# Tiles that straddle two batches take the three-pass path, and w_out2 is split earlier on GpSimd

## The chip, the cores and the metric

The kernel runs on one core of a Trainium2 chip. The metric is device time in microseconds for one execution of the whole program.

## What is computed

A packed attention feeds two feed-forward layers. In the reference, cut to what matters:

```python
# q, k, v: (8, 8, 576, 64), p: (8, 8, 32, 64)
p_packed = sm_attn(p, k, v)                  # 32 packed rows per head
x = sm_attn(q, p_packed, p_packed)           # -> (4608, 512): tokens by head features

h = x @ w_in                                 # (4608, 1024)
sm = softmax(h)
solu = h * sm
ln = (solu - mean(solu)) / sqrt(var(solu) + 1e-6) * g_ln
x = ln @ w_out                               # (4608, 512)

h = maximum(maximum(x @ w1, x @ w2), x @ w3) # (4608, 768)
out = h @ w_out2                             # (4608, 512)
```

## The kernel before

The work runs in three stages, and TensorE's instructions stand in one hand-written order.

**Attention (batches 0 to 7).** For each batch b the kernel forms two things in place of x: the attention weights of the 576 tokens over the packed rows (a, 128 rows for each of two groups of heads), and the packed values already multiplied by w_in (merged, 128 rows by 1024 for each of the two groups). From batch 2 on both are stored to DRAM by GpSimd (m_dram, a_dram; semaphores m_stored and a_stored) and come back later through SP (load_in).

**Stage one (blocks t = 0 to 8 of four tiles of 128 tokens).** Tile n = 4t + i is up(t, i): h = a^T x merged, two halves of 512 columns. 576 is 4.5 tiles, so two batches share nine tiles, and the tiles n = 4, 13, 22 and 31 straddle two batches. The even batch lies in m_even and a_even, the odd one in m_odd and a_odd, each as a pair hi and lo in the format fp32r; the product is three matmuls (PASSES: hi x lo, hi x hi, lo x hi) in `three_passes`, line 783. ScalarE writes hi (hi_in), VectorE lo (lo_in, which counts in_split). `split_after` says after which tile the halves of each batch are made: batch 3 after tile 10, batch 5 after tile 19, batch 7 after tile 28. The slots hold zeros beside the tokens of their batch, so that a straddling tile may be a sum over both. Tile 4 is computed in that way.

The straddling tiles 13, 22 and 31 are computed otherwise: SP loads both batches' merged values and the 64 tokens that each contributes, unsplit, into straddle_m and straddle_a (`load_straddle`), and up issues plain float32 matmuls (line 990), 64 columns of weights each, into the upper or the lower half of the output's partitions. These two tensors lie in the memory of w_out2_s.

A block on TensorE (solu_block) is: up(t,0), up(t,1), down(t-1,0), down(t-1,1), up(t,2), up(t,3), down(t-1,2), down(t-1,3), then four turn_h (transposes, line 1073). down is ln @ w_out, 24 matmuls each, also at line 783. VectorE takes the row maximum, the product and the moments; ScalarE the exponential and the hi parts ln_hi; VectorE writes ln_lo with four subtractions (`lo_t`, line 1574), and up(t+1, 0) waits for the first of them. `block_scale(t)` on GpSimd turns the moments of a block into scales (scale_ready); VectorE's moments of block t + 1 wait for it ahead of a reciprocal, since they overwrite its input.

GpSimd's queue also holds the preparation of the last stage's weights. `split_operands(s)`, nine of them, takes pieces of w1, w2, w3 out of weight_raw (two buffers), forms sums, splits all into hi and lo and stores them to DRAM (w_dram, semaphores w_stored). How many follow block_scale(t) is written out, for t = 0 to 7:

```python
for _ in range((0, 1, 2, 1, 2, 2, 1, 0)[t]):
```

w_out2 is split by GpSimd in three pieces (`split_w_out2`, lines 607 and 609) behind block_scale(7), once tile 31 is done (h_filled at 32), because straddle_m and straddle_a use its place until then.

**Stage two.** 4.5 double blocks of nine groups (lines 1171 and 1194) with operands from DRAM in a ring of three slots, and an output product with w_out2 (line 1203). SP issues load_slot(0) only behind store_y(7), w_stored of all nine pieces, and w_out2_split at 3.

Of the kernel before, what the change touches and what calls it, by code (L numbers as in the profile page):

```python
# [20 lines left out]
P = 128  # L21
# [12 lines left out]
DM = H * D  # L34
# [36 lines left out]
def packed_attention_ffn(nc, q, k, v, p, w_in, w_out, g_ln, w1, w2, w3, w_out2, out):  # L71
# [44 lines left out]
    ln_base = cursor[0]  # L116
    ln = place_split("ln", [P, K1, BLK])
    w_out2_s = place_split("w_out2_s", [P, K2, DM])
    straddle_m = place_at(cursor[0] - 2 * K2 * DM * 4, "straddle_m", [P, 2, QUADS, FF1])
    straddle_a = place_at(cursor[0] - 2 * K2 * DM * 4 + 2 * QUADS * FF1 * 4, "straddle_a", [P, 2, QUADS, TAIL])  # L120
    y_raw_base = cursor[0]
    y_raw = place("y_raw", [P, 2, 2, BLK])
    u_base = cursor[0]
# [120 lines left out]
    a_hi, a_low = sem("a_hi"), sem("a_low")  # L244
    m_stored, a_stored = sem("m_stored"), sem("a_stored")
    in_loaded = [sem(f"in_loaded{i}") for i in range(2)]
    straddle_loaded, w_out2_loaded = sem("straddle_loaded"), [sem(f"w_out2_loaded{i}") for i in range(2)]
    w_out2_hi, w_out2_split = sem("w_out2_hi"), sem("w_out2_split")
    in_hi, in_split = sem("in_hi"), sem("in_split")
    packed_first, packed_second = sem("packed_first"), sem("packed_second")  # L250
    gain_loaded, minus_half_ready = sem("gain_loaded"), sem("minus_half_ready")
# [34 lines left out]
    w_out_v = w_out.rearrange("(k p) n -> p k n", p=P)  # L286
    w_out2_v = w_out2.rearrange("(k p) n -> p k n", p=P)
    thirds = [w.rearrange("(k p) (m i n) -> p k m i n", p=P, m=2, n=P) for w in (w1, w2, w3)]
    def raw_operands(n):
        return weight_raw[n % 2][:, :].rearrange("p (o k n) -> p o k n", o=4, n=P)  # L290

    def raw_count(n):
        return 32 * (n // 2 + 1)

    def rows(t):
        return t.rearrange("b (h g) (p j) d -> b (g p) h (j d)", g=QUADS, j=J)
# [126 lines left out]
    with block:  # L423

        @block.sync
        def _(sp):
# [35 lines left out]
                sp.dma_start(a_s[b % 2][:, 1, :, first:first + S].bitcast(F32), a_dram[b])\  # L462
                    .then_inc(in_loaded[b % 2], 16)

            def load_straddle(q):

                if q > 1:
                    sp.wait_ge(h_filled, 9 * (q - 1) + 5)
                for x in range(2):
                    at = slice(S - TAIL, S) if x == 0 else slice(0, TAIL)  # L470
                    sp.dma_start(straddle_m[:, x, :, :], m_dram[2 * q + x]).then_inc(straddle_loaded, 16)
                    sp.dma_start(straddle_a[:, x, :, :], a_dram[2 * q + x][:, :, at]).then_inc(straddle_loaded, 16)

            load_k(0)
            load_p(0)
            load_k(1)
# [48 lines left out]

            for t in range(6):
                load_in(t + 2)
                if t == 0:
                    sp.wait_ge(m_stored, 16 * (B - 2))
                    sp.wait_ge(a_stored, 16 * (B - 2))  # L530
                    load_straddle(1)
                elif t in (3, 5):
                    load_straddle((t + 1) // 2)
                store_y(t)
                if t == 1:

                    sp.wait_ge(y_stored, 32)
                    sp.wait_ge(m_stored, 16 * (B - 2))
                    load_y(0, 0)
# [2 lines left out]

            sp.wait_ge(w_stored[0], 16 * GROUPS)
            sp.wait_ge(w_stored[1], 16 * GROUPS)
            sp.wait_ge(w_out2_split, K2 // 2)
            load_slot(0)
            sp.wait_ge(y_split, Y_PARTS)
            load_y(0, 1)
# [32 lines left out]
        def _(pool):  # L581
# [7 lines left out]
                           allow_slow_non_contiguous=True).then_inc(gain_loaded, 16)  # L589
            wait_alone(pool, gain_loaded, 16)  # L590

            def load_operands(n):
                i, w = divmod(n, 3)
                dst = weight_raw[n % 2][:, :].rearrange("p (m k n) -> p m k n", m=2, n=P)
                for m in range(2):
                    pool.dma_start(dst[:, 1 - m, :, :], thirds[w][:, :, m, i, :]).then_inc(raw_loaded[n % 2], 16)

            def load_w_out2(n):
                dst = weight_raw[n % 2][:, :].rearrange("p (k n) -> p k n", k=2)
                pool.dma_start(dst, w_out2_v[:, 2 * n:2 * n + 2, :]).then_inc(w_out2_loaded[n % 2], 16)  # L600

            def split_w_out2(n):

                hi, low = (w[:, 2 * n:2 * n + 2, :] for w in w_out2_s)
                raw = weight_raw[n % 2][:, :].rearrange("p (k n) -> p k n", k=2)
                wait_alone(pool, w_out2_loaded[n % 2], 16 * (n // 2 + 1))
                pool.tensor_scalar(hi, raw, 1.0, None, ALU.mult).then_inc(w_out2_hi, 1)
                wait_alone(pool, w_out2_hi, n + 1)
                pool.tensor_tensor(low, raw, hi.bitcast(F32), ALU.subtract).then_inc(w_out2_split, 1)

            def split_operands(s):

                n = s
                raw = raw_operands(n)
                wait_alone(pool, raw_loaded[n % 2], raw_count(n))

                def add(k, c, a, b, op, value):
                    if value:
                        pool.wait_ge(sums_step, value)
                    pool.tensor_tensor(sums[:, c, :, :], a, b, op).then_inc(sums_step, 1)  # L620

                add(0, 0, raw[:, A21], raw[:, A22], ALU.add, 4 * s)
                add(1, 2, raw[:, A11], raw[:, A21], ALU.subtract, 0)
                add(2, 1, sums[:, 0, :, :], raw[:, A11], ALU.subtract, 4 * s + 1)
                add(3, 3, raw[:, A12], sums[:, 1, :, :], ALU.subtract, 4 * s + 3)

                if s > 0:

                    pool.wait_ge(w_stored[0], 16 * s)
                pool.tensor_scalar(stage[:, 0:4, 0, :, :], raw, 1.0, None, ALU.mult).then_inc(weight_hi, 1)  # L630
                pool.wait_ge(weight_hi, n + 1)
                pool.tensor_tensor(stage[:, 0:4, 1, :, :], raw, stage[:, 0:4, 0, :, :].bitcast(F32), ALU.subtract)\
                    .then_inc(weight_split, 1)
                wait_alone(pool, weight_split, n + 1)
                pool.dma_start(w_dram[s][:, 0:4], stage[:, 0:4, :, :, :].bitcast(F32)).then_inc(w_stored[0], 16)
                if n + 2 < GROUPS:

                    load_operands(n + 2)
                pool.wait_ge(sums_step, 4 * s + 4)
                if s > 0:  # L640

                    pool.wait_ge(w_stored[1], 16 * s)
                pool.tensor_scalar(stage[:, 4:8, 0, :, :], sums[:, :, :, :], 1.0, None, ALU.mult).then_inc(sums_hi, 1)
                pool.wait_ge(sums_hi, s + 1)
                pool.tensor_tensor(stage[:, 4:8, 1, :, :], sums[:, :, :, :], stage[:, 4:8, 0, :, :].bitcast(F32),
                                   ALU.subtract).then_inc(sums_split, 1)
                pool.wait_ge(sums_split, s + 1)
                pool.dma_start(w_dram[s][:, 4:8], stage[:, 4:8, :, :, :].bitcast(F32)).then_inc(w_stored[1], 16)
# [101 lines left out]
            store_merged(B - 1)  # L750
            store_weights(B - 1)
            for n in range(2):
                load_operands(n)
            block_scale(0)
            s = 0
            for t in range(1, BLOCKS - 1):
                block_scale(t)
                if t == BLOCKS - 2:
                    for n in range(2):
                        load_w_out2(n)  # L760

                    wait_alone(pool, h_filled, 9 * 3 + 5)
                    for n in range(K2 // 2):
                        split_w_out2(n)
                        if n + 2 < K2 // 2:
                            wait_alone(pool, w_out2_split, n + 1)
                            load_w_out2(n + 2)
                for _ in range((0, 1, 2, 1, 2, 2, 1, 0)[t]):
                    split_operands(s)
                    s += 1  # L770
            block_scale(BLOCKS - 1)


        @block.tensor
        def _(pe):
# [178 lines left out]
            def up(t, i):  # L954
# [2 lines left out]
                terms = tile_terms(n)  # L957

                batch = 2 * (n // 9) + terms[-1][0]
                if n > 9 and len(terms) > 1:  # L960
                    pe.wait_ge(straddle_loaded, 64 * (n // 9))
                elif batch < 2:
                    for low_ready in m_low:
                        pe.wait_ge(low_ready, batch + 1)
                    pe.wait_ge(a_low, batch + 1)
                else:
                    pe.wait_ge(in_split, 2 * (batch - 1))
# [14 lines left out]
                else:  # L982

                    pe.wait_ge(h_used, TPB * t + i - 1)
                if n > 9 and len(terms) > 1:

                    for g in range(QUADS):
                        for w in range(WIDE):
                            for x in range(2):
                                last = pe.matmul(ps[half(x), bank + w, :], straddle_a[:, x, g, :],  # L990
                                                 straddle_m[:, x, g, w * 512:(w + 1) * 512],
                                                 start=g == 0, stop=g == QUADS - 1)
                    last.then_inc(h_filled, 1)
                    return
                three_passes([(ps[:, bank + w, :],
                               [([a_s[slot][:, e, g, at] for e in range(2)],
                                 [m_s[slot][:, e, g, w * 512:(w + 1) * 512] for e in range(2)])
# [211 lines left out]
            def outputs(t, tiles):  # L1209
# [3 lines left out]
                base = 4 * MH * t  # L1213

                pe.wait_ge(h2_split, base + parts * (MH - 1))
                if t == 0:
                    pe.wait_ge(w_out2_split, K2 // 2)
                if t < FOUR:

                    pe.wait_ge(c12_ready, GROUPS * (t + 1) - 1)  # L1220
# [788 lines left out]
```

## Time and profile before

| | |
|---|---|
| median of 3 runs | 1022.33 us (1021.81 to 1023.21) |
| profiled execution | 1022.33 us, its span 1020.5 us |
| TensorE (PE) busy | 993.5 us |
| VectorE (DVE) busy | 594.0 us |
| ScalarE (ACT) busy | 356.0 us |
| GpSimd (POOL) busy | 269.4 us |

The span is the time from the first to the last instruction in the trace. PE are matmuls, PEld loads of weights, which overlap them; SPq is SyncE's queue of DMA issues. Matmuls are pipelined: a single one is recorded as longer than the distance to the next one's start, so durations of matmuls aren't added up, and starts are compared instead. L783 is line 783 of the kernel; `ps` is PSUM, where all matmuls write.

### The profile page before, as it was taken

The numbers are of one execution on the slowest core, as the hardware profiler recorded it, in microseconds if no ns is written. First come the engines' busy times: TensorE is split into PE (matmuls) and PEld (weight loads), VectorE is DVE, ScalarE is ACT, GpSimd is POOL, SyncE is SP. The second block draws the span as 40 slices with busy tenths as digits, with TensorE's granted clock in tenths as the row PEclk, the third lists the DMA queues.
The fourth block names the chain that finished last, engine by engine and source line by source line (L and its number), as shares of the span: only waits on it lengthen the run. The fifth ranks groups of instructions, "written<-read, shape, count | busy, mean of one in ns | idle before, by whom it ended". The sixth has DMA issues, their size and how long they took to land.

```text
span 1020.5 us, 14952 instructions
## 1 busy us (share of the span) xinstructions
PE 993.5 (97%) x6026; PEld 796.6 (78%) x6026; DVE 594.0 (58%) x960; ACT 356.0 (35%) x583; POOL 269.4 (26%) x228
## 2 busy tenths in 40 slices
PE   6989999999999999999999999999999999999998
PEld 5656567887887887878888888888888888888887
DVE  1788899765865767564655726664365736553121
ACT  5867753333442442333212422224122332122111
POOL 0368753439949992700000000000000000000000
PEclk9999999999999999999999999999999999999999
DMA  8979827226564582235745345453544535432341
GB/s 296 390 259 307 295 102 258 106 103 250 216 224 182 193 317 83 103 113 187 295 161 203 134 176 192 174 212 114 196 175 185 179 131 214 163 140 93 117 161 42
DMA packets 49764, 189.85 MB, mean 186 GB/s; under 512 B 9888, under 2 KB 9888, under 8 KB 39328
## 3 DMA queue, kind: packets, MB, share of 16 engines
q1 hardware_dynamic: 43472, 153.89, 42.4%
q0 software_dynamic: 6224, 35.00, 9.1%
q8 instruction: 48, 0.79, 0.3%
q14 instruction: 20, 0.16, 0.1%
HBM read 141.30 MB, written 47.58 MB: 185 GB/s over the span
## 4 chain that ended last, share of the span: by engine, by line
PE 84%; DVE 8%; ACT 4%; issue 3%; DMA 1%; POOL 0%; SPq 0%; ACTq 0%
PE ps L1171 28%; PE ps L783 27%; PE ps L1203 14%; PE ps L1194 5%; PE ps L1073 3%; PE ps L894 2%; DVE h_lo L1574 1%; PE ps L990 1%; DVE spot L1889 1%; PE ps L797 1%; DVE spot L1880 1%; DMA p_raw<-in_p_dram 1%; PE ps L799 1%; DVE a2T L1662 1%; ACT qT L1248 1%
## 5 line engine op out<-in xcount | busy, mean ns | idle before, releaser
L1171 PE MATMUL ps<-ys,slot 128*128 128x512 f32 x1512 | 345.8, 390 | 0.6
L1171 PEld LDWEIGHTS ps<-ys,slot 128*128 128x128 f32 x1512 | 283.2, 188 | 62.5 <-ACT spot L1248 4.0
L1880 DVE TENSOR_TENSOR spot<-ps,spot 128x512 f32<-128x512 f32 x108 | 74.3, 688 | 104.6 <-PE ps L1171 75.1
L1248 ACT ACTIVATE spot<-ps 128x512 f32<-128x512 f32 x90 | 52.8, 597 | 207.9 <-PE ps L1171 196.8
L783 PE MATMUL ps<-ln_lo,w_out_s_hi 128*128 128x512 f32 x280 | 109.2, 390 | 0.0
L783 PE MATMUL ps<-ln_hi,w_out_s_lo 128*128 128x512 f32 x280 | 109.0, 389 | 0.0
L783 PE MATMUL ps<-ln_hi,w_out_s_hi 128*128 128x512 f32 x280 | 108.9, 389 | 0.0
L1203 PE MATMUL ps<-w_out_s_lo,h_hi 128*128 128x512 f32 x216 | 84.0, 389 | 0.0
L1203 PE MATMUL ps<-w_out_s_hi,h_hi 128*128 128x512 f32 x216 | 84.0, 389 | 0.0
L1203 PE MATMUL ps<-w_out_s_hi,h_lo 128*128 128x512 f32 x216 | 84.0, 389 | 0.0
L1390 ACT ACTIVATE u<-ps,neg_max 128x1024 f32<-128x1024 f32 x36 | 40.2, 1117 | 112.7 <-DVE neg_max L1737 112.7
L1248 ACT ACTIVATE h_hi<-spot 128x512 fp32r<-128x512 f32 x54 | 33.8, 633 | 118.4 <-DVE spot L1889 87.3
L1745 DVE TENSOR_TENSOR u<-ps,u 128x1024 f32<-128x1024 f32 x36 | 43.9, 1219 | 38.4 <-ACT u L1390 38.4
L783 PEld LDWEIGHTS ps<-ln_lo,w_out_s_hi 128*128 128x128 f32 x280 | 52.6, 188 | 12.5 <-issue 1.6
L1735 DVE TENSOR_REDUCE row_max<-ps 128x1 f32<-128x1024 f32 x36 | 43.7, 1213 | 30.2 <-PE ps L783 23.9
L783 PEld LDWEIGHTS ps<-ln_hi,w_out_s_lo 128*128 128x128 f32 x280 | 52.6, 188 | 11.0
L783 PEld LDWEIGHTS ps<-ln_hi,w_out_s_hi 128*128 128x128 f32 x280 | 52.6, 188 | 10.8
L1889 DVE TENSOR_TENSOR spot<-ps,spot 128x512 f32<-128x512 f32 x24 | 16.6, 692 | 76.1 <-PE ps L1171 76.1
L1574 DVE TENSOR_TENSOR ln_lo<-ps,ln_hi 128x1024 fp32r<-128x1024 f32 x36 | 41.7, 1216 | 24.0 <-ACT ln_hi L1248 23.8
L1248 ACT ACTIVATE yst<-ps 128x512 f32<-128x512 f32 x36 | 21.4, 596 | 83.0 <-PE ps L783 83.0
L783 PE MATMUL ps<-m_even,a_even 128*128 128x512 f32 x204 | 48.9, 392 | 0.2 <-ACT merged_last L1248 0.2
L1194 PE MATMUL ps<-ys,slot 128*128 128x512 f32 x216 | 49.1, 389 | 0.0
(160 smaller groups left out, 1504.0 us busy)
## 6 DMA issues: line engine op xcount, KB each, us to landing
slot<-w_operands SPq DMA_DIRECT2D x36, 1792.0 KB, 7.2
w_operands<-stage POOLq DMA_DIRECT2D x18, 1024.0 KB, 4.9
v_raw<-in_v_dram SPq DMA_DIRECT2D x8, 1152.0 KB, 7.1
q_raw<-in_q_dram SPq DMA_DIRECT2D x32, 288.0 KB, 5.3
y_features<-yst SPq DMA_DIRECT2D x9, 1024.0 KB, 4.8
y_raw<-y_features SPq DMA_DIRECT2D x9, 1024.0 KB, 5.2
out_dram<-spot SPq DMA_DIRECT2D x36, 256.0 KB, 2.0
slot<-w_operands SPq DMA_DIRECT2D x9, 1024.0 KB, 5.1
```

The lines of the kernel that those rows point to most:

```text
L783: last = pe.matmul(dst, w[a], x[z], start=start and c == 0 and e == 0, stop=stop and c == n - 1 and e == len(PASSES) - 1)
L1073: last = pe.transpose(ps[:, bank + c // 4, (c % 4) * P:(c % 4 + 1) * P], u[:, i, c * P:(c + 1) * P], ident[:, :])
L1171: last = pe.matmul(ps[:, group_bank(g, k), :], w[:, a - 1, i, kk, :], ys[:, b, j, kk, :], start=n < 4 and kk == 0 and e == 0, stop=kk == K ...
L1194: last = pe.matmul(ps[:, group_bank(g, k), :], w[:, a, i, kk, :], ys[:, b, j, kk, :], start=h == 0 and kk == 0 and e == 0, stop=h == 1 and ...
L1203: last = pe.matmul(ps[:, out_bank(n), :], h2[a][:, c, j * P:(j + 1) * P], w_out2_s[z][:, c, :], start=(c == 0 and e == 0), stop=(c == K2 - ...
L1248: return act.activation(dst, src, ACT.Copy)
L1390: act.activation(u[:, i, :].rearrange("r (n c) -> r n c", n=WIDE), ps[:, bank:bank + WIDE, :], ACT.Exp, bias=neg_max[:, i:i + 1], accum_ou ...
L1574: return dve.tensor_tensor(dst, src, hi.bitcast(F32), ALU.subtract)
L1735: dve.tensor_reduce(row_max[:, c], ps[:, bank:bank + WIDE, :], AX.XY, ALU.max).then_inc(h_max, 1)
L1745: dve.tensor_tensor(u[:, i, :].rearrange("r (n c) -> r n c", n=WIDE), ps[:, bank:bank + WIDE, :], u[:, i, :].rearrange("r (n c) -> r n c", ...
L1880: dve.tensor_tensor(dst[:, :], a, b, op).then_inc(ready, 1)
L1889: dve.tensor_tensor(best[m][c][:, :], src, best[m][c][:, :], ALU.max).then_inc(ready, 1)
```

## The change

Tiles 13, 22 and 31 go through `three_passes` with both slots, as tile 4 does; load_straddle, its tensors, its semaphore and its twelve DMAs go. They then wait for in_split of the odd batch. With the place of w_out2_s free once the attention is done, w_out2's three pieces come first in one list with the operands of the last stage: `load_piece` and `split_piece`, right behind block_scale(0) on GpSimd, ahead of all split_operands. The buffers of weight_raw alternate through the whole list; the counts of raw_loaded, weight_hi and weight_split go on from the pieces to the operands. The nine split_operands are spread otherwise over the blocks, and the waits for w_out2_split on SP and TensorE are gone.

```diff
     def raw_count(n):
-        return 32 * (n // 2 + 1)
+        return sum(16 if c < W2_END else 32 for c in range(n % 2, n + 1, 2))
...
             for t in range(6):
                 load_in(t + 2)
-                if t == 0:
-                    sp.wait_ge(m_stored, 16 * (B - 2))
-                    sp.wait_ge(a_stored, 16 * (B - 2))
-                    load_straddle(1)
-                elif t in (3, 5):
-                    load_straddle((t + 1) // 2)
                 store_y(t)
...
             sp.wait_ge(w_stored[1], 16 * GROUPS)
-            sp.wait_ge(w_out2_split, K2 // 2)
             load_slot(0)
...
+            def load_piece(n):
+                if n < W2_END:
+                    src, parts, _, _ = pieces[n]
+                    dst = weight_raw[n % 2][:, :].rearrange("p (k n) -> p k n", k=parts)
+                    pool.dma_start(dst, src).then_inc(raw_loaded[n % 2], 16)
+                    return
+                i, w = divmod(n - W2_END, 3)
...
+            def split_piece(n):
+
+                _, parts, hi, lo = pieces[n]
+                raw = weight_raw[n % 2][:, :].rearrange("p (k n) -> p k n", k=parts)
+                wait_alone(pool, raw_loaded[n % 2], 16 * (n // 2 + 1))
+                pool.tensor_scalar(hi, raw, 1.0, None, ALU.mult).then_inc(weight_hi, 1)
+                wait_alone(pool, weight_hi, n + 1)
+                pool.tensor_tensor(lo, raw, hi.bitcast(F32), ALU.subtract).then_inc(weight_split, 1)
+
+                wait_alone(pool, weight_split, n + 1)
+                load_piece(n + 2)
...
             for n in range(2):
-                load_operands(n)
+                load_piece(n)
             block_scale(0)
+
+            wait_alone(pool, a_stored, 16 * (B - 2))
+            wait_alone(pool, m_stored, 16 * (B - 2))
+            wait_alone(pool, t_filled, 1)
+            for n in range(W2_END):
+                split_piece(n)
             s = 0
-            for t in range(1, BLOCKS - 1):
+            for t in range(1, BLOCKS):
                 block_scale(t)
-                if t == BLOCKS - 2:
-                    for n in range(2):
-                        load_w_out2(n)
-
-                    wait_alone(pool, h_filled, 9 * 3 + 5)
-                    for n in range(K2 // 2):
-                        split_w_out2(n)
-                        if n + 2 < K2 // 2:
-                            wait_alone(pool, w_out2_split, n + 1)
-                            load_w_out2(n + 2)
-                for _ in range((0, 1, 2, 1, 2, 2, 1, 0)[t]):
+                for _ in range((0, 1, 2, 1, 1, 2, 1, 1, 0)[t]):
                     split_operands(s)
                     s += 1
-            block_scale(BLOCKS - 1)
...
-                if n > 9 and len(terms) > 1:
-                    pe.wait_ge(straddle_loaded, 64 * (n // 9))
-                elif batch < 2:
+                if batch < 2:
...
-                if n > 9 and len(terms) > 1:
-
-                    for g in range(QUADS):
-                        for w in range(WIDE):
-                            for x in range(2):
-                                last = pe.matmul(ps[half(x), bank + w, :], straddle_a[:, x, g, :],
-                                                 straddle_m[:, x, g, w * 512:(w + 1) * 512],
-                                                 start=g == 0, stop=g == QUADS - 1)
-                    last.then_inc(h_filled, 1)
-                    return
```

## Rows read from the trace of the kernel before

**Rows 1.** The page: TensorE's busy time, and the chain by engine.

```profile
PE 993.5 (97%) x6026; PEld 796.6 (78%) x6026; DVE 594.0 (58%) x960; ACT 356.0 (35%) x583; POOL 269.4 (26%) x228
...
PE 84%; DVE 8%; ACT 4%; issue 3%; DMA 1%; POOL 0%; SPq 0%; ACTq 0%
```

**Rows 2.** The chain in order of time: start us, us, what.

```profile
195.24 32.75 PE ps L783 x144
...
234.33 3.58 PE ps L990 x16
...
397.88 3.58 PE ps L990 x16
```

**Rows 3.** Windows: stretch, length, busy us (and count) by engine, clock, DMA.

```profile
195.24:231.49 36.25, 36.25 (x178) 30.52 (x178) 24.25 (x39) 13.74 (x19) 17.87 (x18) 1.00 0.40 148
231.49:268.84 37.35, 37.35 (x181) 29.23 (x181) 25.35 (x39) 13.74 (x19) 35.24 (x29) 1.00 0.65 235
...
448.84:475.70 26.86, 25.53 (x129) 21.54 (x128) 18.17 (x24) 13.77 (x20) 0.00 (x0) 1.00 0.57 215
475.70:1020.50 544.80, 540.98 (x2377) 444.99 (x2375) 262.30 (x404) 135.24 (x219) 0.00 (x0) 1.00 0.46 165
```

**Rows 4.** TensorE's waits, first 150 to 450 us, then 450 to 500 us.

```profile
PE ps L1073 <- DVE u L1745: 1.5, 1, 1.5
...
PE ps L1085 <- ACT ln_hi L1248: 1.3, 1, 1.3
```

**Rows 5.** Timeline of TensorE: start us, us, instruction; three separate stretches.

```profile
147.15 7.05 PE L783 MATMUL ps<-m_even,a_even 128*128 128x512 f32 x30 [0.22 <-ACT merged_last L1248]
...
158.12 1.04 PE L1073 MATMUL ps<-ident,u 128*128 128x128 f32 x8
...
175.26 5.60 PE L783 MATMUL ps<-m_odd,a_odd 128*128 128x512 f32 x24
180.70 0.39 PE L783 MATMUL ps<-ln_lo,w_out_s_hi 128*128 128x512 f32 x1
...
234.26 3.65 PE L990 MATMUL ps<-straddle_m,straddle_a 128*64 128x512 f32 x16
...
237.85 0.50 PE L783 MATMUL ps<-ln_lo,w_out_s_hi 128*128 128x512 f32 x1
```

**Rows 6.** Timeline of GpSimd, and the page's row of its stores (us to landing).

```profile
176.09 0.20 POOL L742 TENSOR_TENSOR late_scale<-inv_std,inv_sum 128x4 f32<-128x4 f32 x1
192.55 0.20 POOL L734 TENSOR_TENSOR inv_sq<-inv_sum 128x4 f32<-128x4 f32 x1 [16.26 <-DVE mean_var L1763]
...
375.07 1.42 POOL L620 TENSOR_TENSOR sums<-weight_raw 128x256 f32<-128x256 f32 x2
...
387.10 2.97 POOL L645 TENSOR_TENSOR stage<-sums,stage 128x1024 fp32r<-128x1024 f32 x1
390.36 0.60 POOL L648 DMA_DIRECT2D w_operands<-stage  x1 [0.30 <-POOL stage L645]
...
415.29 2.79 POOL L607 TENSOR_SCALAR w_out_s_hi<-weight_raw 128x1024 fp32r<-128x1024 f32 x1 [2.63 <-DMA weight_raw<-in_moe_w_out_dram]
...
429.79 2.39 POOL L609 TENSOR_TENSOR w_out_s_lo<-weight_raw,w_out_s_hi 128x1024 fp32r<-128x1024 f32 x1
...
w_operands<-stage POOLq DMA_DIRECT2D x18, 1024.0 KB, 4.9
```

**Rows 7.** Timeline of VectorE: splits of batches 2, 3 and 7, and ln_lo.

```profile
182.01 2.28 DVE L1574 TENSOR_TENSOR m_even<-m_even 128x2048 fp32r<-128x2048 f32 x1
...
193.72 4.62 DVE L1574 TENSOR_TENSOR ln_lo<-ps,ln_hi 128x1024 fp32r<-128x1024 f32 x4 [1.25 <-ACT ln_hi L1248]
...
220.45 1.35 DVE L1574 TENSOR_TENSOR a_odd<-a_odd 128x1152 fp32r<-128x1152 f32 x1
...
387.73 3.55 DVE L1574 TENSOR_TENSOR a_odd<-a_odd 128x1152 fp32r<-128x1152 f32 x1
```

**Rows 8.** Timeline of SP's queue.

```profile
450.12 0.56 SPq L517 DMA_DIRECT2D slot<-w_operands  x1
```

More of the change, by code:

```diff
@@ L118, in packed_attention_ffn @@
     w_out2_s = place_split("w_out2_s", [P, K2, DM])
-    straddle_m = place_at(cursor[0] - 2 * K2 * DM * 4, "straddle_m", [P, 2, QUADS, FF1])
-    straddle_a = place_at(cursor[0] - 2 * K2 * DM * 4 + 2 * QUADS * FF1 * 4, "straddle_a", [P, 2, QUADS, TAIL])
     y_raw_base = cursor[0]
@@ L246, in packed_attention_ffn @@
     in_loaded = [sem(f"in_loaded{i}") for i in range(2)]
-    straddle_loaded, w_out2_loaded = sem("straddle_loaded"), [sem(f"w_out2_loaded{i}") for i in range(2)]
-    w_out2_hi, w_out2_split = sem("w_out2_hi"), sem("w_out2_split")
     in_hi, in_split = sem("in_hi"), sem("in_split")
@@ L288, in packed_attention_ffn @@
     thirds = [w.rearrange("(k p) (m i n) -> p k m i n", p=P, m=2, n=P) for w in (w1, w2, w3)]
+    pieces = []
+    for c in range(0, K2, 2):
+        pieces.append((w_out2_v[:, c:c + 2, :], 2, w_out2_s[0][:, c:c + 2, :], w_out2_s[1][:, c:c + 2, :]))
+    W2_END = len(pieces)
     def raw_operands(n):
@@ L463, in load_in @@
                     .then_inc(in_loaded[b % 2], 16)
-            def load_straddle(q):
-                if q > 1:
-                    sp.wait_ge(h_filled, 9 * (q - 1) + 5)
-                for x in range(2):
-                    at = slice(S - TAIL, S) if x == 0 else slice(0, TAIL)
-                    sp.dma_start(straddle_m[:, x, :, :], m_dram[2 * q + x]).then_inc(straddle_loaded, 16)
-                    sp.dma_start(straddle_a[:, x, :, :], a_dram[2 * q + x][:, :, at]).then_inc(straddle_loaded, 16)
             load_k(0)
@@ L590, in _ @@
             wait_alone(pool, gain_loaded, 16)
-            def load_operands(n):
-                i, w = divmod(n, 3)
+            def load_piece(n):
[5 more added lines that the diff above has]
+                i, w = divmod(n - W2_END, 3)
                 dst = weight_raw[n % 2][:, :].rearrange("p (m k n) -> p m k n", m=2, n=P)
@@ L596, in load_operands @@
                     pool.dma_start(dst[:, 1 - m, :, :], thirds[w][:, :, m, i, :]).then_inc(raw_loaded[n % 2], 16)
[L598 to L609, printed above, removed]
+            def split_piece(n):
[7 more added lines that the diff above has]
+                load_piece(n + 2)
             def split_operands(s):
-                n = s
+                n = W2_END + s
                 raw = raw_operands(n)
@@ L635, in split_operands @@
                 pool.dma_start(w_dram[s][:, 0:4], stage[:, 0:4, :, :, :].bitcast(F32)).then_inc(w_stored[0], 16)
-                if n + 2 < GROUPS:
-                    load_operands(n + 2)
+                if n + 2 < W2_END + GROUPS:
+                    load_piece(n + 2)
                 pool.wait_ge(sums_step, 4 * s + 4)
@@ L984, in up @@
                     pe.wait_ge(h_used, TPB * t + i - 1)
-                if n > 9 and len(terms) > 1:
-                    for g in range(QUADS):
-                        for w in range(WIDE):
-                            for x in range(2):
-                                last = pe.matmul(ps[half(x), bank + w, :], straddle_a[:, x, g, :],
-                                                 straddle_m[:, x, g, w * 512:(w + 1) * 512],
-                                                 start=g == 0, stop=g == QUADS - 1)
-                    last.then_inc(h_filled, 1)
-                    return
                 three_passes([(ps[:, bank + w, :],
@@ L1215, in outputs @@
                 pe.wait_ge(h2_split, base + parts * (MH - 1))
-                if t == 0:
-                    pe.wait_ge(w_out2_split, K2 // 2)
                 if t < FOUR:
```

## The prediction

> **What bounds the kernel now.** I read the page's busy line and chain first. TensorE is busy for 97% of the span and carries 84% of the chain that ended last [rows 1], so TensorE's own work is the first suspect. Then the chain in order of time: from 195 us on, where the diff's mixed tiles lie, it is one unbroken run of TensorE pieces: matmuls of L783 and the mixed tiles at L990, 3.58 us each, three in all (first and last in [rows 2]). The windows cut at the block borders say the same: a block without an L990 tile is 36.25 us long with TensorE busy for 36.25 of it, the first one with such a tile is 37.35 long and busy for 37.35 [rows 3]. TensorE's waits from 150 to 450 us are a single one of 1.5 us, before any of the three tiles, and from 450 to 500 us a single one of 1.3 us, on ScalarE's ln_hi [rows 4]. So in this stretch each microsecond put on TensorE should be one on the end, and work on any other engine costs nothing until it makes TensorE wait. The granted clock is 1.00 in all these windows [rows 3], the 2.4 GHz level, with TensorE already busy throughout; more of the same matmuls gives no row a reason to change it.
>
> **The three mixed tiles (n = 13, 22, 31): what goes.** L990 issues eight plain float32 matmuls with 64 columns of weights, which the trace shows as 16 records. From the first of them to the first matmul of the next piece is 237.85 - 234.26 = 3.59 us [rows 5]. Their gaps also count, so I take the price from the blocks. Four tiles of 12 matmuls and four down-projections of 24 are 144 matmuls; they take 32.75 us [rows 2], 0.2274 us per matmul, start to start. A block with the L990 tile has 132 of these, so the tile's price including its drains is 37.35 - (36.25 - 12 x 0.2274) = 37.35 - 33.52 = 3.83 us.
>
> **What comes.** The tile now takes the three-pass path: 2 column halves x 2 batches x 2 groups of heads x 3 passes = 24 matmuls of 128x512 in fp32r. That is 24 x 0.2274 = 5.46 us. Two rows check it. A run of 24 starts at 175.26 and its follower at 180.70: 5.44 us. And tile n = 4 already goes this very way, switching between m_even and m_odd: it is the second half of the 48 matmuls from 147.15 to 158.12, 10.97 us, 0.2285 each [rows 5], so 5.44 to 5.49 us. Net +5.46 - 3.83 = +1.63 us a tile, **+4.9 us for three**. As bounds: without the drains (3.59 us) the difference is 1.87, +5.6 us for three; if the new tile ran at the quickest pitch, 5.44 against 3.83, 1.61, +4.8 us. I take 4.9, since the block windows hold the gaps at both ends.
>
> A page speaks of this price too. Rows: a pair of float32 matmuls into the two halves of the output takes 3.59 / 4 = 0.90 us, four times the 0.2274 us of an fp32r one. The Trainium skill (FP8 and Floating Point Precision, TensorE Precision Notes) gives true FP32 four passes through the array, and the Trainium skill (TensorEngine Tiling (Array Packing), Key Properties) lets tiles of the array run in parallel; the trace agrees with both together. By the four passes alone the eight would be 8 x 0.91 = 7.3 us and the change would save time, which is the opposite answer; by the row it costs.
>
> **New waits of these tiles.** They now need in_split of the odd batch, the split of inputs on VectorE, instead of straddle_loaded. For tile 13 the split ends at 220.45 + 1.35 = 221.80, the tile starts at 234.26: 12 us of slack. Tile 31 is the tightest: the split ends at 387.73 + 3.55 = 391.28 and the tile starts at 397.88 [rows 2, 7], 6.6 us. Tile 22's split lies at the end of the block before. All move with TensorE when it gets later, so these waits cost 0; behind them on TensorE stand the down-projections, which would pay every microsecond if the slack were used. Loads into the even slot still wait for the mixed tile's h_filled and start about 1.6 us later, with a block and more until they are read.
>
> **SP's queue.** Twelve loads go, six of them of 1 MB each by the tile's shape. No wait of TensorE ends in them, so their going gives 0. Before load_slot(0), SP loses its wait on w_out2_split, but store_y(7) stands ahead of it in the queue and load_slot(0) was issued only at 450.12 [rows 8], 18 us after the last w_out2 split ended at 429.79 + 2.39 = 432.18 [rows 6]; gain 0.
>
> **GpSimd.** The three w_out2 splits with their loads move from block 7 to just behind block_scale(0), whose last instruction runs at 176.09. There GpSimd was idle until 192.55 [rows 6]. The three took 415.29 to 432.18 = 16.9 us with one load issued among them; now each of the three is followed by the issue of piece n + 2, so I allow 19 us: done at about 195 to 197. The waits ahead of them (stores of the last merged and weight tiles, first transpose) name things issued ahead of block_scale(0), and weight_raw's first loads are issued there too, before a pause in which GpSimd waits for block 0's moments: 0. Queued behind is block_scale(1), due at 192.55, so up to 4 us late. Who waits for it is VectorE's reciprocal in moments(2, 0), which comes only after the four ln_lo of block 1, at 193.72 + 4.62 = 198.3 [rows 7], and after a max, an exponential and a product: covered. Then the nine split_operands: one takes 375.07 to 390.36 + 0.60 = 15.9 us without its load's issue, 17 with it. The new order takes one from block 4 and puts it in block 7, in the place of the 16.9 us of w_out2, so GpSimd still ends near 433 + 5 = 438 us; its last store follows, with 4.9 us to landing for such a one [rows 6], and the first reader, load_slot(0), comes at about 450.1 + 4.9 = 455. That leaves some 12 us of slack: 0. If GpSimd got later by more than that, each further microsecond would delay the slot load and could then reach group 0.
>
> **The one place where the move can hurt** is VectorE in block 1. At 387.10 GpSimd's L645 (2.97 us) and VectorE's L1574 on a_odd met, and the latter took 3.55 us instead of 1.35 [rows 6, 7]: 2.2 us lost. Now GpSimd works from 176 on, where VectorE splits batch 2 from 182.01. VectorE was idle for 1.25 us ahead of its ln_lo at 193.72, so that much is free; TensorE starts up(2, 0) at 195.24, and it needs the first ln_lo, over at 193.72 + 4.62 / 4 = 194.9, 0.3 us more. One such collision therefore costs 2.2 - 1.25 - 0.3 = 0.6 us, none costs 0. I take 0: the split starts while GpSimd, by the sum above, is issuing the load behind piece 0 (176.3 + 2.8 + 2.4 + 0.3 = 181.8), and a lesser meeting fits into 1.25. The Trainium skill (SBUF — State Buffer, SBUF: two separate sides) calls this an exclusive lock on ports shared by the two engines; the 3.55 us row agrees, and the sum doesn't use it.
>
> **Sum.** The profiled execution took 1022.33 us, of which 1020.5 span, and is itself the median of the three runs. 1022.33 + 4.9 + 0 + 0 = **1027.2 us**, +0.48%. Against 0.2%, 2.0 us, which is about what a measurement of this kernel can tell from no change, that is more than twice as much.
>
> **Rivals.**
> (a) *Collision in block 1*: VectorE's batch-2 split waits for a GpSimd instruction, TensorE stalls at up(2, 0), once. For it: the 3.55 us row. Against it: the idle time in front of ln_lo. 1027.2 + 0.6 = 1027.8 us, 0.08.
> (b) *Part comes back at the joint to stage two*: TensorE's idle 26.86 - 25.53 = 1.3 us between 448.84 and 475.70 [rows 3] vanishes, if ScalarE's ln_hi is there sooner for some reason of the new order. 1025.9 us, still slower. Against it: the wait is for ScalarE, which TensorE itself releases. 0.04.
> (c) *The extra is absorbed*: the later stage is paced by slot loads or VectorE and TensorE's idle there takes it up. Idle after 448.84 is 1.3 + (544.80 - 540.98 = 3.8) = 5.1 us [rows 3], enough for 4.9, giving 1022.3. Against it: no wait is named there beyond 1.3 us, and a wait for another engine would have to be one whose time doesn't depend on TensorE. 0.05.
> (d) *The other side*: the two half-width streams at L990 do not truly run side by side, and the price is the four passes of each of the eight matmuls, 8 x 4 x 0.2274 = 7.3 us. Then each tile saves 1.8, and the kernel ends at 1022.3 - 5.5 = 1016.8 us. It decides as soon as the L990 tile costs more than 5.46 us. Speaking for it: 16 records for eight instructions, so they are split up somehow; against it, strongly, the 3.59 us and the block lengths. This is also the four-pass rule of the Trainium skill (FP8 and Floating Point Precision, TensorE Precision Notes) taken by itself. 0.04.
>
> **How the numbers follow.** The forecast has 0.79, and with (a) and (b) slower holds 0.91; (c) gives same 0.05, (d) faster 0.04. The range holds the forecast with its bounds +4.8 to +5.6 (1027.1 to 1027.9), (a) added to the upper bound (1028.5), and (b) below (1025.9); runs of before spread from 1021.81 to 1023.21, so I put half a microsecond outside below and 0.3 above: 1025.4 to 1028.8. (c) and (d), 0.09, stay out.
>
> **What would show it.** Blocks 3, 5 and 7 at about 39.0 us instead of 37.35, all others still 36.25; matmuls of L783 on m_even and m_odd up by 36 each, L990 gone; TensorE's waits unchanged from 150 to 500 us; group 0 starting near 475.7 + 4.9 = 480.6. GpSimd full from 176 to about 196, with block_scale(1) a few microseconds late and nobody waiting. Wrong would be: a new TensorE wait on VectorE's split ahead of a mixed tile or of up(2, 0); GpSimd still splitting after 450; or stage two shorter than 544.8 us, which would be (c).

## The result

The changed kernel takes 1030.66 us (median of 6 runs, 1029.28 to 1030.95), the kernel before 1023.31 us (6 runs, 1021.81 to 1023.49): a ratio of 1.0072, 95% interval 1.0061 to 1.0082. It is slower by 7.35 us where 4.9 were forecast, and lies above the range. The direction and its largest term were right; a second term, forecast at 0, is 2.4 us.

The profiled execution has a span of 1029.3 us, 8.8 more than [rows 1] belong to. The chain in order of time (start us, us, what) shows where two parts of that are:

```profile
199.01 32.93 PE ps L768 x144
231.94 3.50 PE ps L1046 x32
235.44 35.49 PE ps L768 x156
...
310.66 35.48 PE ps L768 x156
...
385.88 35.48 PE ps L768 x156
```

L768 is the old L783, L1046 the old L1073, and L990 is gone: blocks 3, 5 and 7 now have one run of 156 matmuls. But block 2, which started at 195.24 in [rows 2], starts at 199.01, before any of the three tiles. The windows at the block borders (columns as in [rows 3]):

```profile
199.01:235.44 36.43, 36.43 (x177) 30.67 (x178) 24.40 (x39) 12.55 (x17) 19.95 (x22) 1.00 0.41 148
235.44:274.42 38.98, 38.98 (x189) 32.75 (x189) 24.27 (x39) 13.73 (x19) 36.87 (x31) 1.00 0.63 231
274.42:310.66 36.24, 36.24 (x177) 30.51 (x178) 24.20 (x39) 13.74 (x19) 20.78 (x18) 1.00 0.41 148
...
484.47:1029.30 544.83, 541.02 (x2377) 444.98 (x2375) 262.23 (x404) 135.10 (x219) 0.00 (x0) 1.00 0.46 165
```

A block with a straddling tile is 38.98 us against 37.35 [rows 3], +1.63, three times 4.9; a plain one and stage two (544.83 against 544.80) are as before, with the clock at 1.00 throughout. TensorE's timeline tells the rest:

```profile
163.03 2.98 PE L768 MATMUL ps<-m_odd,a_odd 128*128 128x512 f32 x12
...
194.83 2.81 PE L1046 MATMUL ps<-ident,u 128*128 128x128 f32 x24 [0.73 <-DVE u L1716]
199.01 3.00 PE L768 MATMUL ps<-m_odd,a_odd 128*128 128x512 f32 x12 [1.36 <-DVE ln_lo L1545]
```

The same two pieces of m_odd in the kernel before:

```profile
161.53 2.99 PE L783 MATMUL ps<-m_odd,a_odd 128*128 128x512 f32 x12
...
195.09 2.98 PE L783 MATMUL ps<-m_odd,a_odd 128*128 128x512 f32 x12
```

From the first matmul of such a piece to the first of block 2 it takes 199.01 - 163.03 = 35.98 us; before, 195.09 - 161.53 = 33.56. (The chain in [rows 2] has 195.24 there, since it lets a piece begin where the transposes before it end.) That is 2.42 us in block 1, with two waits for VectorE, 0.73 and 1.36 us, that [rows 4] don't have. The three tiles' 4.9 and these 2.4 make 7.3 us, the difference of the medians but for rounding. The remaining 1.5 us of the spans' difference lie ahead of 163 us, where the two programs issue the same to TensorE. The profiled executions of the ten variants below start that piece anywhere between 161.1 and 163.9 us, so this is the spread between executions.

VectorE and GpSimd in that place, from their timelines (VectorE first):

```profile
182.38 1.22 DVE L1716 TENSOR_TENSOR u<-ps,u 128x1024 f32<-128x1024 f32 x1 [1.27 <-ACT u L1361]
183.52 3.87 DVE L1545 TENSOR_TENSOR m_even<-m_even 128x2048 fp32r<-128x2048 f32 x1
187.31 3.55 DVE L1545 TENSOR_TENSOR a_even<-a_even 128x1152 fp32r<-128x1152 f32 x1
...
197.69 4.56 DVE L1545 TENSOR_TENSOR ln_lo<-ps,ln_hi 128x1024 fp32r<-128x1024 f32 x4
```

```profile
180.64 2.40 POOL L596 TENSOR_TENSOR w_out_s_lo<-weight_raw,w_out_s_hi 128x1024 fp32r<-128x1024 f32 x1
183.34 0.81 POOL L582 DMA_DIRECT2D weight_raw<-in_moe_w_out_dram  x1 [0.30 <-POOL w_out_s_lo L596]
184.18 2.81 POOL L594 TENSOR_SCALAR w_out_s_hi<-weight_raw 128x1024 fp32r<-128x1024 f32 x1
187.07 2.57 POOL L596 TENSOR_TENSOR w_out_s_lo<-weight_raw,w_out_s_hi 128x1024 fp32r<-128x1024 f32 x1
```

VectorE's split of batch 2 was 2.28 us for m_even [rows 7] and 1.35 for an undisturbed a; now it is 3.87 and 3.55, 3.8 us more. The idle 1.25 us ahead of ln_lo in [rows 7] is used up, and ln_lo comes late for TensorE.

### The profile page after: what moved, and what is told of

Same layout as the page of the kernel before. It is cut to its first block, busy times and chain, and to the rows that moved or that the text cites. A ratio compares the mean times of both kernels' runs of the same rounds, so it can differ in the third digit from the quotient of the medians.

```text
span 1029.3 us, 14988 instructions
## 1 busy us (share of the span) xinstructions
PE 1001.0 (97%) x6050; PEld 808.6 (79%) x6050; DVE 598.8 (58%) x960; ACT 355.9 (35%) x583; POOL 269.2 (26%) x228
## 4 chain that ended last, share of the span: by engine, by line
PE 82%; DVE 11%; ACT 4%; issue 3%; DMA 0%; POOL 0%; ACTq 0%; DVEq 0%
PE ps L1144 28%; PE ps L768 25%; PE ps L1176 14%; PE ps L1167 5%; PE ps L1046 2%; PE ps L879 2%; PE ps L782 1%; DVE h_lo L1545 1%; DVE spot L1860 1%; DVE bn L1726 1%; PE ps L828 1%; DVE spot L1851 1%; ACT a1T L1219 1%; PE ps L784 1%; ACT qT L1219 1%
## 5 line engine op out<-in xcount | busy, mean ns | idle before, releaser
L1144 PE MATMUL ps<-ys,slot 128*128 128x512 f32 x1512 | 345.8, 390 | 0.5
L768 PE MATMUL ps<-ln_hi,w_out_s_lo 128*128 128x512 f32 x280 | 109.0, 389 | 0.0
L768 PE MATMUL ps<-ln_lo,w_out_s_hi 128*128 128x512 f32 x280 | 108.9, 389 | 0.0
L768 PE MATMUL ps<-ln_hi,w_out_s_hi 128*128 128x512 f32 x280 | 108.9, 389 | 0.0
L768 PEld LDWEIGHTS ps<-ln_lo,w_out_s_hi 128*128 128x128 f32 x280 | 52.6, 188 | 11.1
L768 PEld LDWEIGHTS ps<-ln_hi,w_out_s_hi 128*128 128x128 f32 x280 | 52.6, 188 | 10.9
L768 PEld LDWEIGHTS ps<-ln_hi,w_out_s_lo 128*128 128x128 f32 x280 | 52.5, 188 | 10.9
L768 PE MATMUL ps<-m_odd,a_odd 128*128 128x512 f32 x240 | 57.7, 391 | 1.4 <-DVE ln_lo L1545 1.4
L768 PE MATMUL ps<-m_even,a_even 128*128 128x512 f32 x240 | 57.8, 392 | 0.2 <-ACT merged_last L1219 0.2
L768 PEld LDWEIGHTS ps<-m_odd,a_odd 128*128 128x128 f32 x240 | 44.7, 188 | 10.8 <-issue 1.6
```

The source lines that it names most:

```text
L768: last = pe.matmul(dst, w[a], x[z], start=start and c == 0 and e == 0, stop=stop and c == n - 1 and e == len(PASSES) - 1)
L1144: last = pe.matmul(ps[:, group_bank(g, k), :], w[:, a - 1, i, kk, :], ys[:, b, j, kk, :], start=n < 4 and kk == 0 and e == 0, stop=kk == K ...
```

## The experiments

Each ran in turns with the kernel before; the medians of before lay between 1022.4 and 1023.4 us in the four sets, so the ratios count. (The quotient of the two medians can differ from the ratio by up to 0.07%, within its interval.) e1 to e4 test where the 7.35 us come from; e5 to e8 what a meeting of the two engines costs; e9 and e10 a detail left open by those.

The profiled executions, one of each, tell the variants apart more finely than the medians, if the spread ahead of block 1 is left out. On TensorE, in us:

| | start of the piece of m_odd | from it to block 2 | from it to the end of the span | more than before |
|---|---|---|---|---|
| before | 161.53 | 33.56 | 859.0 | |
| changed | 163.03 | 35.98 | 866.3 | 7.3 |
| e1 | 163.30 | 33.55 | 863.9 | 4.9 |
| e2 | 162.92 | 35.98 | 861.4 | 2.4 |
| e3 | 161.21 | 33.57 | 859.0 | 0.0 |
| e4 | 162.73 | 33.55 | 863.8 | 4.8 |
| e5 | 162.52 | 33.60 | 863.8 | 4.8 |
| e6 | 162.64 | 33.57 | 863.8 | 4.8 |
| e7 | 163.88 | 33.76 | 864.0 | 5.0 |
| e8 | 161.10 | 34.38 | 864.6 | 5.6 |
| e9 | 161.98 | 33.63 | 863.9 | 4.9 |
| e10 | 163.61 | 33.58 | 863.9 | 4.9 |

**e1: GpSimd held until batch 2 is split, and respaced.**

```diff
             wait_alone(pool, t_filled, 1)
+            wait_alone(pool, in_split, 2)
             for n in range(W2_END):
...
-                for _ in range((0, 1, 2, 1, 1, 2, 1, 1, 0)[t]):
+                for _ in range((0, 0, 2, 1, 2, 2, 1, 1, 0)[t]):
```

> The changed kernel, but GpSimd waits for VectorE's split of batch 2 to be over (in_split at 2) before the first w_out2 piece, and the split_operands are spread (0, 0, 2, 1, 2, 2, 1, 1, 0), so that GpSimd also pauses during VectorE's split of batch 3. Nothing of the computation is left out. Theory: of the 7.35 us that the changed kernel lost, 4.9 are the three tiles (their blocks measure 38.98 us against 37.35) and 2.5 are one collision of the two engines in block 1, where m_even took 3.87 us instead of 2.28 and a_even 3.55 instead of 1.35. Then this kernel takes 1023.3 + 4.9 = 1028.2 us, m_even of batch 2 is back at 2.28 and a_even at 1.35, and TensorE's waits of 1.4 us for ln_lo and 0.7 us for u are gone. Rival: the 2.5 us come from elsewhere (the attention stage, which was 1.5 us longer in the profiled run, or the changed DMA traffic): then it stays at about 1030.6 us though the collision is gone.

Measured: 1027.76 us, ratio 1.0045 (1.0031 to 1.0058), by the ratio +4.6 us. VectorE's timeline:

```profile
183.79 2.28 DVE L1546 TENSOR_TENSOR m_even<-m_even 128x2048 fp32r<-128x2048 f32 x1
185.99 1.35 DVE L1546 TENSOR_TENSOR a_even<-a_even 128x1152 fp32r<-128x1152 f32 x1
195.48 4.62 DVE L1546 TENSOR_TENSOR ln_lo<-ps,ln_hi 128x1024 fp32r<-128x1024 f32 x4 [1.23 <-ACT ln_hi L1220]
```

The split and the idle 1.23 us are back, and TensorE doesn't wait at either place any more. The collision is the second term; what is left is the tiles' 4.9.

**e2: the three tiles in their old form.**

```diff
+                if n > 9 and len(terms) > 1:
+                    for g in range(QUADS):
+                        for w in range(WIDE):
+                            for x in range(2):
+                                at = slice(S - TAIL, S) if x == 0 else slice(TAIL, 2 * TAIL)
+                                last = pe.matmul(ps[half(x), bank + w, :], a_s[x][:, 0, g, at].bitcast(F32),
+                                                 m_s[x][:, 0, g, w * 512:(w + 1) * 512].bitcast(F32),
+                                                 start=g == 0, stop=g == QUADS - 1)
+                    last.then_inc(h_filled, 1)
+                    return
```

> The changed kernel with everything as it is, but tiles 13, 22 and 31 as eight plain float32 matmuls of 64 columns of weights each, as before, now read from the hi parts in the slots; the lo parts are left out for these tiles. Theory: each of the three blocks is 37.35 us again and the kernel takes 1030.7 - 4.9 = 1025.8 us, of which 2.5 us over the kernel before are the collision. Rival that blames the tiles for everything (7.35 us, 2.45 a tile): 1023.3 us.

Measured: 1026.01 us, ratio 1.0028 (1.0017 to 1.0038), by the ratio +2.9 us. The chain has the old tile back, at its old price:

```profile
235.32 2.83 PE ps L768 x12
238.15 3.58 PE ps L973 x16
241.73 27.43 PE ps L768 x120
```

while m_even still takes 3.85 us and a_even 3.55. The rival that blames the tiles for all of it expected a ratio of 1.000 and is out.

**e3: both edits together.**

> Both edits in one: GpSimd held until batch 2 is split, with the spread (0, 0, 2, 1, 2, 2, 1, 1, 0), and the three tiles as float32 matmuls on the hi parts (lo parts left out for these tiles). What is left of the change is the missing twelve loads and waits on SP, and w_out2 split early. Theory: these are worth nothing, so it takes what the kernel before does, 1023.3 us, within 0.7. Rival: the missing loads or the earlier place of w_out2 are worth something by themselves, either way: over 1 us away from 1023.3.

Measured: 1023.20 us, ratio 1.0002 (0.9992 to 1.0011). Twelve loads fewer and w_out2 split 230 us earlier are worth nothing that can be measured, as forecast.

**e4: only piece 1 held** (`if n == 1: wait_alone(pool, in_split, 2)` ahead of its TENSOR_SCALAR).

> The changed kernel, but only piece 1 of w_out2 waits for VectorE's split of batch 2; piece 0 and the issue of the load behind it stay where they were, so that only that DMA issue (183.34 to 184.15 in the changed kernel's trace) meets m_even (from 183.52). Nothing is left out. Theory A, the compute instructions of GpSimd block VectorE, an issue doesn't: m_even 2.28 us, a_even 1.35. Theory B, the issue blocks it as well: m_even 2.28 + 0.6 = 2.9 us, a_even 1.35. In both the delay is under the 1.25 us of idle time ahead of ln_lo, so both expect 1028.2 us, like the kernel that holds all three pieces, if block_scale(1) being some microseconds later doesn't matter; if it does (VectorE's reciprocal of block 2 waits for it), up to 2 us more.

Measured: 1027.04 us, ratio 1.0045 (1.0029 to 1.0061). The issue ran from 183.05 to 183.86, m_even from 183.22 in 2.28 us: an issue alone doesn't slow it (theory A). Holding one piece is enough.

**e5: the hold without the respacing.**

> As the kernel that held all three pieces behind VectorE's split of batch 2, but with the changed kernel's own spread of split_operands (one behind block_scale(1)). Nothing is left out. Theory: the collision only moves. GpSimd's work runs on into block 2, where its TENSOR_SCALAR and TENSOR_TENSOR for the sums (some 220 to 225 us) meet VectorE's split of batch 3 (m_odd from 220.0, a_odd from 222.2 where it was undisturbed). Then m_odd or a_odd takes 1.5 to 4 us more than 2.28 and 1.35 in sum, and TensorE stalls at the start of block 3 by that less 1.6: 1028.5 to 1030.6 us. Rival: only block 1 is sensitive, 1027.4 us, the median of the kernel that held and respaced.

Measured: 1027.59 us, ratio 1.0048 (1.0035 to 1.0061). GpSimd did meet the split of batch 3, but the theory's size was wrong:

```profile
219.28 2.28 DVE L1546 TENSOR_TENSOR m_odd<-m_odd 128x2048 fp32r<-128x2048 f32 x1
221.47 2.19 DVE L1546 TENSOR_TENSOR a_odd<-a_odd 128x1152 fp32r<-128x1152 f32 x1
230.99 4.62 DVE L1546 TENSOR_TENSOR ln_lo<-ps,ln_hi 128x1024 fp32r<-128x1024 f32 x4 [0.41 <-ACT ln_hi L1220]
```

0.84 us lost, and the idle time ahead of ln_lo fell from 1.25 to 0.41: all of it absorbed. Here GpSimd's TENSOR_SCALAR at 220.48 was the one to wait (3.72 us instead of 2.8).

**e6: piece 1's TENSOR_SCALAR starts with a_even** (`in_split` at 1 in place of 2).

> The changed kernel, but piece 1's TENSOR_SCALAR waits until VectorE has finished m_even of batch 2, so it starts with a_even, and its TENSOR_TENSOR comes when VectorE is past the split. Nothing is left out. What is open: how much a TENSOR_SCALAR of GpSimd costs a two-input instruction of VectorE that starts with it. If it is held for the whole 2.8 us, a_even takes 1.35 + 2.8 = 4.2 us; if only for its first part, as with a_even at 351.47 in the kernel before (2.19 us), 2.2 us. m_even is 2.28. The delay of 0.9 us is under the idle time, time 1027.4; that of 2.8 would give a stall of 1.2 and 1028.6.

Measured: 1027.80 us, ratio 1.0046 (1.0033 to 1.0060). Neither of the two expectations: a_even stayed at 1.35 us and the TENSOR_SCALAR, 0.25 us later in its start, took 3.73.

**e7: piece 1's TENSOR_TENSOR held** (`in_split` at 2 ahead of it; the TENSOR_SCALAR as in the changed kernel).

> The changed kernel, but piece 1's TENSOR_TENSOR waits until VectorE's split of batch 2 is over; its TENSOR_SCALAR starts 0.66 us into m_even as in the changed kernel. Nothing is left out. Theory of two separate collisions: m_even is still 3.87 us, a_even is back at 1.35, the delay is 1.6 in place of 3.8, all but nothing of it reaches TensorE, and the time is 1027.4 to 1027.7 us. Rival: the 3.87 us belong to the TENSOR_TENSOR too, both back to normal, same time; the trace tells these apart.

Measured: 1028.41 us, ratio 1.0055 (1.0043 to 1.0068):

```profile
184.37 3.86 DVE L1547 TENSOR_TENSOR m_even<-m_even 128x2048 fp32r<-128x2048 f32 x1
188.15 1.35 DVE L1547 TENSOR_TENSOR a_even<-a_even 128x1152 fp32r<-128x1152 f32 x1
196.32 4.57 DVE L1547 TENSOR_TENSOR ln_lo<-ps,ln_hi 128x1024 fp32r<-128x1024 f32 x4
```

So there are two meetings, each with its own price: 1.6 us on m_even from the TENSOR_SCALAR, 2.2 on a_even from the TENSOR_TENSOR. With the first alone the idle time is used up and TensorE starts block 2 only 0.2 us late (33.76 us against 33.56) instead of 2.4. By its median this kernel lies above the forecast for it; the interval takes in the 1.0048 of e5.

**e8: piece 0's TENSOR_TENSOR starts with m_even** (`h_used` at 7 ahead of it).

> The changed kernel, but piece 0's TENSOR_TENSOR waits for the product of tile 6 on VectorE (h_used at 7), the instruction right before m_even, so both start together. Nothing is left out. If one of the two has to wait for the whole of the other, either m_even takes 2.28 + 2.3 = 4.6 us or the TENSOR_TENSOR 2.40 + 2.2 = 4.6. In the first case the following TENSOR_SCALAR meets a_even as well, the delay is 3 us or more and TensorE stalls by 1.5 or more: 1029 us or more; in the second VectorE loses at most 1 us and the time is 1027.4.

Measured: 1028.88 us, ratio 1.0056 (1.0043 to 1.0069). VectorE, then GpSimd:

```profile
181.58 2.28 DVE L1547 TENSOR_TENSOR m_even<-m_even 128x2048 fp32r<-128x2048 f32 x1
183.78 3.56 DVE L1547 TENSOR_TENSOR a_even<-a_even 128x1152 fp32r<-128x1152 f32 x1
...
194.17 4.57 DVE L1547 TENSOR_TENSOR ln_lo<-ps,ln_hi 128x1024 fp32r<-128x1024 f32 x4
```

```profile
181.81 4.30 POOL L598 TENSOR_TENSOR w_out_s_lo<-weight_raw,w_out_s_hi 128x1024 fp32r<-128x1024 f32 x1 [3.20 <-DVE u L1718]
```

The first to start kept its time, and the waiting one went next, ahead of a_even. One collision of 2.2 us, and TensorE waited 0.66 us for ln_lo and starts block 2 0.8 us late: about the 0.6 us that rival (a) gave for exactly this.

**e9 and e10: the same TENSOR_SCALAR early in m_even, but with no DMA issue right ahead of it** (e10 has a small fill of GpSimd more; in e9 the loop is over range(0)):

```diff
+                if n == 1:
+                    wait_alone(pool, h_used, 7)
+                    for f in range(1):
+                        pool.memset(late_scale[:, TPB * 8:], 0.0).then_inc(filler, 1)
+                        wait_alone(pool, filler, f + 1)
                 pool.tensor_scalar(hi, raw, 1.0, None, ALU.mult).then_inc(weight_hi, 1)
+                if n == 1:
+                    load_piece(2)
...
-                load_piece(n + 2)
+                if n > 0:
+                    load_piece(n + 2)
```

> The changed kernel, but piece 1's TENSOR_SCALAR waits for the product ahead of m_even (h_used at 7) and starts some 0.25 us into m_even, and the load of piece 2 is issued behind it instead of ahead of it. Nothing is left out. Open is why m_even lost 1.6 us to a TENSOR_SCALAR that started 0.65 us into it and wasn't itself slowed (2.81 us), while in three other meetings the TENSOR_SCALAR waited and the VectorE instruction in flight kept its time. Theory O, the one in flight keeps the lock: m_even 2.28 us, TENSOR_SCALAR 2.8 + 1.9 = 4.7 us. Theory P, what matters is that the DMA issue ended right ahead of the TENSOR_SCALAR: the same here, as no issue is near. Theory Q, VectorE can be interrupted in the first part of a long instruction: m_even 3.9 us or so, TENSOR_SCALAR 2.8. The time of the kernel: at most 1028.5, at least 1027 us.

> As the one before, with one small fill of four unused columns of late_scale ahead of the TENSOR_SCALAR, so that it starts some 0.6 us into m_even, the offset of the changed kernel, again with no DMA issue near. Theory P (the issue right ahead matters): m_even 2.28, TENSOR_SCALAR 2.8 + 1.6 = 4.4 us. Theory Q (the early part of a long instruction can be interrupted at this offset): m_even 3.87, TENSOR_SCALAR 2.81 as in the changed kernel.

Measured: e9 1027.31 us, ratio 1.0045 (1.0033 to 1.0057); e10 1028.69 us, ratio 1.0049 (1.0029 to 1.0069). In both m_even is 2.28 us, the TENSOR_SCALAR waits (4.65 and 4.50 us), and a_even loses 0.84. e10's start, 0.42 us into m_even, fell short of the planned 0.6. Theory Q has nothing for it at these offsets. O and P both fit these two; but O doesn't fit the changed kernel, and P, that the issue right ahead matters, does. The offset of the changed kernel, 0.66, wasn't reached without an issue.

e3's trace has the counterpart, an issue right ahead and a small offset, in its block 7 (GpSimd, then VectorE):

```profile
384.79 0.65 POOL L625 DMA_DIRECT2D w_operands<-stage  x1 [0.30 <-POOL stage L622]
385.46 2.80 POOL L633 TENSOR_SCALAR stage<-sums 128x1024 fp32r<-128x1024 f32 x1
```

```profile
385.20 3.48 DVE L1556 TENSOR_TENSOR m_odd<-m_odd 128x2048 fp32r<-128x2048 f32 x1
```

The TENSOR_SCALAR starts 0.26 us into m_odd, as in e9 (0.27), but 0.02 us behind an issue, and m_odd loses 1.20 us where e9's m_even lost nothing. At this offset it is the issue that makes the difference.

## Why the prediction missed, point by point

**The tiles: right.** 5.46 - 3.83 = 1.63 us a tile was forecast, 38.98 - 37.35 = 1.63 measured, three times; e2 gives the old price back. Taking the old price from block lengths instead of the 3.59 us was what made it exact. Rival (d) is out: the old form does cost less than 24 fp32r matmuls.

**In_split, SP's queue, block_scale(1), GpSimd's end: right at 0.** No wait ahead of the three tiles; load_slot(0) was issued at 458.87, after GpSimd's last store at 434.47. GpSimd's new spread also met the splits of batches 6 and 7 otherwise than before, 2.98 and 2.39 us lost against 0.84 and 2.20, which the prediction didn't look at; VectorE was idle for 3.8 and 5.8 us ahead of its ln_lo there even so, and no wait came of it. block_scale(1) came at 198.64, its reader on VectorE at 211.06. Rivals (b) and (c) are out: TensorE is idle between 457.60 and 484.47 for 1.3 us as before, and stage two is as long as before.

**The step that failed** is "I take 0: the split starts while GpSimd, by the sum above, is issuing the load behind piece 0 (...), and a lesser meeting fits into 1.25". The timetable in it was right: m_even did start 0.18 us into the issue. The conclusion wasn't. The issue lasts 0.81 us and the split 3.6, so what counts is what GpSimd runs behind the issue, a TENSOR_SCALAR and a TENSOR_TENSOR. They met both halves of the split, 1.6 + 2.2 = 3.8 us. Rival (a) had the place, the mechanism and the absorbing idle time right, and e8 comes near its 0.6 us for a single meeting (0.8); but it counted one meeting where two fitted, and the range was built on that. Less the absorbed 1.25 and the 0.3 of slack, 3.8 leave 2.25; 2.42 were measured in block 1. The slack was mis-sized too: TensorE's first matmul of block 2 starts 1.32 us after the start of ln_lo when it has waited for it, and 1.37 us after it in the kernel before (195.09 - 193.72), so the slack was 0.05 us and not 0.3. With the prediction's own arithmetic for two meetings the forecast would have been 1022.3 + 4.9 + 2.3 = 1029.5.

**Not settled:** why m_even lost 1.6 us to a TENSOR_SCALAR that started 0.65 us into it (changed kernel, e2, e7) and m_odd 1.20 to one 0.26 us into it (e3), though they had started first. In e5, e6, e8, e9 and e10 the instruction in flight kept its time. In the four slow cases one issue ended 0.02 or 0.03 us ahead of the TENSOR_SCALAR; in e5 two did as well, yet there it started 1.2 us into m_odd and had to wait. So both a near issue and an early offset are needed, or one issue where e5 had two; the runs don't part these. All four slow durations are the offset, 0.93 or 0.94 us, and the full 2.28 again (0.66 + 0.93 + 2.28 = 3.87; 0.26 + 0.94 + 2.28 = 3.48), as if VectorE's instruction had begun anew; that is arithmetic, no run shows what happens inside.

## What to carry to other kernels

Work moved into an engine's idle time is free only if no other engine does something there that it blocks: lay the moved instructions one by one against the neighbour's, and charge each meeting, not the likeliest one. Compare the sum with the idle time ahead of the next consumer, since up to that point it costs nothing (e5, e9) and beyond it nearly all of it shows (2.42 of the 3.8 - 1.25 = 2.5 us in block 1). The two meetings cost VectorE 3.8 us in block 1 and 3.0 in block 6; only block 1 had too little idle time behind them. On an engine that is full, price a swap of instructions from block lengths with and without it.

## What the runs showed of the hardware

Eight float32 matmuls with 64 columns of weights, in pairs to the two halves of the output, took 3.83 us with their gaps, less than 24 fp32r matmuls of full width (5.46).

VectorE's subtraction of two SBUF operands and GpSimd's elementwise instructions of 128x1024 exclude each other, mostly in order of start: a GpSimd TENSOR_TENSOR that came 0.23 us into m_even took 4.30 us instead of 2.40 (e8). The Trainium skill (SBUF — State Buffer, SBUF: two separate sides) says that whichever starts first holds the ports for its whole instruction. The TENSOR_TENSOR meetings agree nearly: one that began 1.14 us ahead of m_even (262.51 us in the kernel before) cost it 1.12, 2.26 of its 2.40 us in sum. The TENSOR_SCALAR ones don't in full. In the changed kernel, VectorE and then GpSimd:

```profile
356.45 3.06 DVE L1545 TENSOR_TENSOR m_even<-m_even 128x2048 fp32r<-128x2048 f32 x1
```

```profile
356.29 2.81 POOL L633 TENSOR_SCALAR stage<-sums 128x1024 fp32r<-128x1024 f32 x1
```

A head start of 0.16 us cost m_even 0.78; one of 0.37 us cost it 0.57 (e2, 353.10), one of 0.74 us cost m_odd 0.20 (392.70), and one of 0.99 us nothing (e2, 389.37). So a TENSOR_SCALAR of 2.8 us held such a subtraction back for some 0.94 us from its own start, and not for 2.8; the 0.84 us of e5, e9 and e10 are of that kind. And in the changed kernel m_even had started first and lost 1.6 us all the same. There the measurements decide. A DMA issue on GpSimd by itself cost VectorE nothing (e4).
